# Summing v in the layout of its products, eight products on ScalarE, and rewritten orders up to the second tile

## The chip, the cores and the metric

One core of one Trainium2 chip. The metric is device time in microseconds of one execution of the whole program, the median of several runs. TensorE (PE) does matmuls and transposes, VectorE (DVE), ScalarE (ACT) and GpSimd (POOL) work on SBUF, SyncE (SP) issues DMAs. Each engine works through its own list in order and waits on semaphores.

## The reference

Inputs are q, k, v of shape (4 batches, 8 heads, 576 positions, 64) in fp32. The attention output is the sum of two parts:

```
pooled: q, k, v averaged over groups of 4 positions (144 rows), softmax attention over the 144, each row repeated 4 times
local:  scores of position i with |i - j| < 4 only (7 taps), softmax, times v
x = (pooled + local), reshaped to 2304 x 512
moe:  xn = x / rms(x) * g;  y = (silu(xn @ w_gate) * (xn @ w_val)) @ w_out      d_ff 1536
moe2: h = y @ w_in;  out = (s * relu(h)^2 + b) @ w_out                          d_ff 2048
```

## The kernel before, in words

The 576 groups of four positions are cut into five tiles `a` (or `t`) of up to 128 partitions; a partition holds four positions (`FAC`).

*Pooled attention* runs once for 4 x 8 = 32 heads `n`, in a pipeline over four engines: TensorE makes the scores (`CSC`, line 1480), VectorE the minimum `cneg` (line 1330; the scores come negated), ScalarE the exponents (`cs`, line 1168), TensorE turns them (line 1491), ScalarE copies them (`cpT`, line 1159), TensorE multiplies them with the summed v (`dv`, line 1513). TensorE works on score n, turn n-2 and product n-3 in one pass of its loop. Between passes it turns the summed q and k of the next batch (`turn_pooled`, line 1468; six units a batch, from the pass `UNIT_FROM` = 5 of the batch before). Their sums over four positions come first: q on VectorE (`pool_q`), k on GpSimd (`pool_k`). For v of batches 1 to 3, VectorE sums it in a layout of 128 partitions with nine rows each (`vd`); SP stores it to DRAM (`store_vd`) and loads it back with 72 partitions as `dv` (`load_dv`). Batch 0's v is already loaded with 72 partitions and summed there (`pool_v0`). `finish_pooled` scales the result by the inverse sum of the exponents, SP stores it (`store_co`) and loads it per tile (`load_ct`).

*Local attention* of a tile has 16 products in each of two phases, two for each head. In the first (`qk_mult`, line 532) GpSimd multiplies q with seven shifted windows of k, 128x896, and VectorE reduces over 64 (`qk_reduce`). After a softmax over seven taps on VectorE and ScalarE comes the second (`pv_mult`, line 546): GpSimd multiplies the probabilities with windows of v, writing with a stride of seven so that the taps lie side by side, and VectorE reduces over seven into `x` (`pv_reduce`). The products go through two buffers `prod`, so GpSimd is at most two products ahead of VectorE. Then the pooled part is added (`add_pooled0`, `add_pooled`), ScalarE squares and sums, VectorE finds the inverse root (Newton's steps), ScalarE scales x.

*First layer.* TensorE transposes x, ScalarE and VectorE split it into a high part, a low part and a bf16 copy (`split_hi`, `split_lo`, `split_bf`). Steps `s` of the layer: steps 0 to 11 are half a tile wide (256 columns), 12 to 17 full (512), together tile 0; then 12 steps for each further tile. A step is gate, value and, two steps later, output, 12 matmuls each, with `silu`, `hidden_mul`, `hidden_hi`, `hidden_lo` between them on ScalarE and VectorE. The weights come in 18 pieces through four buffers: load, high part on ScalarE (`weight_hi`), low part on GpSimd or VectorE (`weight_lo`).

*The order* is written out by hand. In each engine's loop over heads and, later, steps, tables say after which n or s a piece of tile 0's or tile 1's work stands (`QK0_AT`, `PV0_AT`, `SUMQ_AT`, `SUMV_AT`, `QK1_AT`, `PV1_AT`, `HI_AT`, `LO_AT`, `REST_AT`). SP's list of loads is one sequence. From tile 2 on the orders are common to before and after. Step 18 is the first of tile 1; its transposes stand after the output of step 14.

Of the kernel before, what the change touches and what calls it, by code (L numbers as in the profile page):

```python
# [4 lines left out]
F32 = mybir.dt.float32  # L5
# [3 lines left out]
ALU = mybir.AluOpType  # L9
# [61 lines left out]
HI_AT = {0: (6, 7), 2: (8,), 4: (9,), 5: (10,), 6: (11,), 8: (12,), 9: (13,), 10: (14,), 12: (15,), 13: (16,), 14: (17,)}  # L71
LO_AT = {0: (4,), 2: (6,), 4: (8,), 7: (10,), 9: (12,), 11: (14,)}
QK1_AT = {0: (7, 8), 1: (9,), 3: (10, 11), 4: (12,), 5: (13, 14), 6: (15,)}
PV1_AT = {8: (0, 1), 9: (2, 3), 10: (4, 5), 11: (6, 7), 12: (8, 9, 10, 11), 13: (12, 13, 14), 14: (15,)}

REST_AT = {("qk", 7): (5,), ("qk", 10): (7,), ("qk", 15): (9,), ("pv", 3): (11,), ("pv", 6): (13,), ("pv", 15): (15, 17)}

PRODUCTS = [("qk", 0, n) for n in range(16)] + [("pv", 0, n) for n in range(16)] + [("qk", 1, n) for n in range(16)]
# [26 lines left out]
QK_REST = {(1, 9): (2, 3), (1, 10): (4, 5, 6), (1, 11): (7, 8), (2, 0): (9, 10, 11, 12), (2, 1): (13, 14, 15), (3, 0): (13, 14, 15), (4, 0): (13, 14, 15)}  # L105
# [38 lines left out]

def build(nc, q, k, v, w_gate, w_val, w_out, rms_g, w2_in, w2_out, s2, b2, out):
    y_scr = nc.dram_tensor("y_scr", [TILES, P, DT, W_], F32, kind="Internal").ap()
    c_scr = nc.dram_tensor("c_scr", [G, E], F32, kind="Internal").ap()
    v_scr = nc.dram_tensor("v_scr", [B, H * J, D], F32, kind="Internal").ap()

    with ExitStack() as ctx:  # L150
# [81 lines left out]
        rawv = [None] + [place(at, f"rawv{b}", [P, QT, FAC * D], F32) for b in (1, 3)]  # L232
# [9 lines left out]
        rawv = [None, rawv[1], place(at, "rawv2", [P, QT, FAC * D], F32), rawv[2]]  # L242
# [66 lines left out]
        prod_ready, prod_used = sem("prod_ready"), sem("prod_used")  # L309
        shifted, expd, probs = sem("shifted"), sem("expd"), sem("probs")  # L310
# [80 lines left out]
        def weight_hi(act, n):  # L391
# [1185 lines left out]
```

## Time and profile before

| what | us |
|---|---|
| median of 3 runs | 1009.58 (1008.57 to 1010.66) |
| the profiled execution | 1014.44 |
| its span, first to last instruction | 1010.8 |
| busy: TensorE | 957.7 (95%) |
| busy: VectorE | 529.1 (52%) |
| busy: GpSimd | 416.6 (41%) |
| busy: ScalarE | 329.0 (33%) |

Busy shares are averages over stages with different limits: GpSimd has nothing left to do in the last third, and TensorE is not full in the first. The rows below are therefore taken by stage.

### The profile page before, as it was taken

The page shows a single profiled execution, that of the slowest core. Times are in us where ns is not written, and L with a number is a line of the kernel's source. Part 1 is how long each engine was busy: PE and PEld are TensorE (multiplying, and loading weights), DVE is VectorE, ACT ScalarE, POOL GpSimd, SP SyncE. Part 2 cuts the span into 40 slices and gives each one's busy share as a digit, 9 for nine tenths or more (in the row PEclk, how much of TensorE's full clock was granted, in tenths as well). Part 3 has the DMA queues.
Part 4 walks back from the last instruction along what each step waited for, and adds up shares of the span by engine and source line. Part 5 has one row for each costly group of instructions (what it writes and reads, how often), then busy time and mean ns, then how long its engine had stood idle before and what let it go on. Part 6 is the DMA issues. An engine that isn't in the chain of part 4 may idle for free.

```text
span 1010.8 us, 12761 instructions
## 1 busy us (share of the span) xinstructions
PE 957.7 (95%) x4836; PEld 766.2 (76%) x4864; DVE 529.1 (52%) x787; ACT 329.0 (33%) x704; POOL 416.6 (41%) x216
## 2 busy tenths in 40 slices
PE   4398899998999999999999999999999999999997
PEld 3276688966677777777777998888888888888896
DVE  4567878887676576555552223443433443433343
ACT  2244564425322431243123344322222322222232
POOL 4788889898787487555630255100000000000000
PEclk9999999999999999999999999999999999999999
DMA  9986345431422032102103243101001100100010
GB/s 255 276 250 194 102 134 159 151 110 51 137 72 82 21 121 75 41 19 71 32 7 125 83 127 105 42 1 64 21 0 42 42 1 1 63 1 1 0 43 21
DMA packets 54376, 79.38 MB, mean 79 GB/s; under 512 B 9836, under 2 KB 37068, under 8 KB 52908
## 3 DMA queue, kind: packets, MB, share of 16 engines
q1 hardware_dynamic: 53212, 73.86, 24.2%
q10 hardware_dynamic: 1104, 4.72, 1.2%
q8 instruction: 38, 0.62, 0.3%
q14 instruction: 22, 0.18, 0.1%
HBM read 67.05 MB, written 11.50 MB: 78 GB/s over the span
## 4 chain that ended last, share of the span: by engine, by line
PE 78%; POOL 7%; DVE 6%; issue 3%; ACT 2%; DMA 2%; SPq 1%; ACTq 0%; POOLq 0%; DVEq 0%
PE bank L727 23%; PE bank L867 7%; PE bank L868 6%; PE bank L869 6%; PE bank L849 6%; PE bank L850 6%; PE bank L851 6%; PE bank L763 4%; PE bank L761 4%; PE bank L762 4%; POOL prod L532 3%; POOL prod L546 2%; DMA rawk<-in_k_dram 2%; PE bank L1480 1%; DVE sc L552 1%
## 5 line engine op out<-in xcount | busy, mean ns | idle before, releaser
L532 POOL TENSOR_TENSOR prod<-qs,ks 128x896 f32<-128x896 f32 x80 | 177.2, 2238 | 73.4 <-DVE sc L552 61.0
L546 POOL TENSOR_TENSOR prod<-sc,vs 128x896 f32<-128x896 f32 x80 | 151.9, 2011 | 51.9 <-DVE x L562 32.5
L888 DVE SCALAR_TENSOR_TENSOR r<-bank,r 128x512 f32<-128x512 f32 (+1 forms) x80 | 51.0, 638 | 181.0 <-ACT r L876 181.0
L851 PE MATMUL bank<-y_h,w2i_l 128*128 128x512 f32 (+1 forms) x320 | 117.7, 368 | 0.0
L876 ACT ACTIVATE r<-bank 128x512 f32<-128x512 f32 (+1 forms) x80 | 44.4, 555 | 182.0 <-PE bank L851 181.2
L761 PE MATMUL bank<-h_h,wo_h 128*128 128x512 f32 (+1 forms) x264 | 102.7, 389 | 0.0
L552 DVE TENSOR_REDUCE sc<-prod 128x14 f32<-128x896 f32 x80 | 85.3, 1078 | 31.7 <-POOL prod L532 31.7
L783 DVE TENSOR_TENSOR bank<-bank,u 128x512 f32<-128x512 f32 (+1 forms) x66 | 39.5, 599 | 119.0 <-PE bank L727 119.0
L727 PE MATMUL bank<-x_h,wv_h 128*128 128x512 f32 (+1 forms) x264 | 100.4, 392 | 0.0
L562 DVE TENSOR_REDUCE x<-prod 128x128 f32<-128x896 f32 x80 | 85.8, 1079 | 18.0 <-POOL prod L546 17.4
L763 PE MATMUL bank<-h_h,wo_l 128*128 128x512 f32 (+1 forms) x264 | 93.2, 353 | 0.0
L762 PE MATMUL bank<-h_l,wo_h 128*128 128x512 f32 (+1 forms) x264 | 92.5, 350 | 0.0
L727 PE MATMUL bank<-x_l,wv_h 128*128 128x512 f32 (+1 forms) x264 | 90.8, 355 | 0.0
L727 PE MATMUL bank<-x_h,wg_h 128*128 128x512 f32 (+1 forms) x264 | 89.4, 360 | 1.0 <-ACT u L771 0.8
L727 PE MATMUL bank<-x_l,wg_h 128*128 128x512 f32 (+1 forms) x264 | 88.0, 355 | 0.3 <-DVE x_l L705 0.3
L867 PE MATMUL bank<-w2o_ha,g_h 128*128 128x512 f32 x216 | 84.3, 390 | 0.4 <-ACT y_st L797 0.4
L868 PE MATMUL bank<-w2o_la,g_h 128*128 128x512 f32 x216 | 84.2, 390 | 0.0
L869 PE MATMUL bank<-w2o_ha,g_l 128*128 128x512 f32 x216 | 84.0, 389 | 0.0
L882 ACT ACTIVATE g_h<-r 128x512 fp32r<-128x512 f32 (+1 forms) x80 | 47.1, 589 | 101.0 <-DVE r L890 101.0
L896 DVE TENSOR_TENSOR g_l<-r,g_h 128x512 fp32r<-128x512 f32 (+1 forms) x80 | 51.2, 639 | 52.5 <-ACT g_h L882 52.5
L777 ACT ACTIVATE h_h<-bank 128x512 fp32r<-128x512 f32 (+1 forms) x66 | 34.4, 521 | 133.1 <-DVE bank L783 133.1
L771 ACT ACTIVATE u<-bank 128x512 f32<-128x512 f32 (+1 forms) x66 | 34.3, 519 | 129.4 <-PE bank L727 129.3
(131 smaller groups left out, 1911.8 us busy)
## 6 DMA issues: line engine op xcount, KB each, us to landing
raww<-in_moe_w_out_dram SPq DMA_DIRECT2D x14, 512.0 KB, 3.9
ks<-in_k_dram SPq DMA_DIRECT2D x16, 280.0 KB
vs<-in_v_dram SPq DMA_DIRECT2D x16, 280.0 KB, 5.0
y_scr<-y_st ACTq DMA_DIRECT2D x4, 1024.0 KB, 4.0
raww<-in_moe_w_in_dram SPq DMA_DIRECT2D x8, 512.0 KB, 3.8
y_raw<-y_scr SPq DMA_DIRECT2D x4, 1024.0 KB, 4.9
out_dram<-o_st SPq DMA_DIRECT2D x16, 256.0 KB, 2.8
rawq<-in_q_dram SPq DMA_DIRECT2D x3, 1152.0 KB, 14.2
```

The costliest lines, as they stand in the source:

```text
L532: pool.tensor_tensor(dst, qv, kv, ALU.mult).then_inc(prod_ready, 1)
L546: pool.tensor_tensor(dst, pv, vv, ALU.mult).then_inc(prod_ready, 1)
L552: dve.tensor_reduce(sc[:, a % 2, n * 2 * BAND:(n + 1) * 2 * BAND], prod[:, at_ % 2, :].rearrange("p (s d) -> p s d", d=D), op=ALU.add, axi ...
L562: dve.tensor_reduce(x[:, 2 * half:2 * half + 2, h * D:(h + 1) * D], over(prod[:, at_ % 2, :], [[BAND * D, 2], [BAND, D], [1, BAND]]), op=A ...
L727: last = pe.matmul(o[:, 0:w], wt[:, m, kk, :], xs[:, kk, cols], start=i == 0, stop=i == 3 * DT - 1)
L761: pe.matmul(o, wo_h[:, m, cols], h_h[:, s % 3, 0:w], start=m == 0 and p != 1, stop=False)
L762: pe.matmul(o, wo_h[:, m, cols], h_l[:, s % 3, 0:w], start=False, stop=False)
L763: last = pe.matmul(o, wo_l[:, m, cols], h_h[:, s % 3, 0:w], start=False, stop=m == M1 - 1)
L851: last = pe.matmul(o, w2i_l[:, m, kk, :], y_h[t % 2][:, kk, 0:w], start=False, stop=kk == DT - 1)
L867: pe.matmul(o, g_h[:, r % 3, cols], wh[:, mh, :], start=m == 0, stop=False)
L868: pe.matmul(o, g_h[:, r % 3, cols], wl[:, mh, :], start=False, stop=False)
L869: last = pe.matmul(o, g_l[:, r % 3, cols], wh[:, mh, :], start=False, stop=m == M2 - 1)
```

## The change

- v of batches 1 to 3 is loaded in halves of 72 partitions (`load_rawv(b, g)`, three buffers) and summed where it is used, without `v_scr`: batches 1 and 2 on VectorE (`pool_v(b, g)`), batch 3 on GpSimd (`pool_v3(g)`).
- Four second-phase products of tile 0 and four of tile 1 (`ACT_PV`: n = 2, 6, 10, 13) go to ScalarE (`pv_taps`): for each of the product's two positions f seven ACTIVATEs, one a tap, of 128x64 with the probability as the per-partition scale, into a buffer `prod_a` of its own. VectorE reduces them with `pv_reduce_act`.
- `finish_pooled` is cut in two (`exponent_sums` and the scaling); `store_co` goes from SP's list to ScalarE's; `UNIT_FROM` becomes 4 for batches 2 and 3; the transposes of tile 0's second half go from steps 2 and 3 to 4 and 5.
- The orders of SP, GpSimd, VectorE and ScalarE up to step 17 are written as plain sequences. Waits change with the buffers: `weight_hi` of the first two pieces waits for two q sums and one k sum, `weight_lo` of the first four for v's sums, `split_hi` of the first chunk for `pool_v3`.

```diff
-UNIT_FROM = 5
+UNIT_FROM = {1: 5, 2: 4, 3: 4}
+ACT_PV = {0: (2, 6, 10, 13), 1: (2, 6, 10, 13)}
...
+        def pv_taps(act, a, n, f):
+            h, half = divmod(n, 2)
+            if f == 0:
+                act.wait_ge(probs, a + 1)
+                act.wait_ge(v_loaded[slot_of(a, h)], 48 * slot_turn(a, h))
+                wait(act, act_used, act_at(a, n))
+                if a == 1:
+                    act.wait_ge(co_stored, 16 * B)
+            for tap in range(BAND):
+                at_ = (h * FAC + 2 * half + f) * BAND + tap
+                last = act.activation(over(prod_a[a][:, f * BAND * D + tap:], [[BAND, D]]),
+                                      v_win(a, h)[:, (2 * half + f + tap) * D:(2 * half + f + tap + 1) * D],
+                                      ACT.Copy, scale=sc[:, a % 2, at_:at_ + 1])
+            if f == 1:
+                last.then_inc(act_made, 1)
...
+            def pool_v3(g):
+                i = 4 + g
+                rv = rawv[i % 3][0:JH, :, :]
+                pool.wait_ge(rawv_loaded[i % 3], 16 * (i // 3 + 1))
+                pool.wait_ge(cpv, H * (B - 3) + 4 * g + 4)
+                pool.tensor_tensor(rv[:, :, 0:2 * D], rv[:, :, 0:2 * D], rv[:, :, 2 * D:4 * D], ALU.add).then_inc(v_order, 1)
+                pool.wait_ge(v_order, g + 1)
+                pool.tensor_tensor(dv[0:JH, (B - 1) % 2, H * g:H * (g + 1), :], rv[:, :, 0:D], rv[:, :, D:2 * D], ALU.add).then_inc(v3_pooled, 1)
...
```

SP's new list, calls only, up to the second weight piece:

```
rawk0, rawq0 in thirds, load_rawv0(0), load_qk(0,0), load_rawq(1), load_qk(0,1), load_rawk(1), load_rawv0(1),
load_qk(0,2), load_rawv(1,0), load_qk(0,4), load_rawv(1,1), load_qk(0,3), load_rawq(2), load_rawk(2), load_qk(0,5),
load_rawv(2,0), load_v(0,0), load_qk(0,7), load_qk(0,6), small constants, load_rawv(3,0), load_rawq(3), load_rawk(3),
load_piece(0), load_v(0,1), load_rawv(2,1), load_rawv(3,1), load_qk(1,0), load_v(0,2), (0,4), (0,3), (0,5), load_ct(0), load_piece(1)
```

GpSimd's new list: `qk_mult(0, 0..3)`, `pool_k(1)`, `qk_mult(0, 4..9)`, `pool_k(2)`, `qk_mult(0, 10..15)`, `pool_v3(0)`, `pool_k(3)`, the `pv_mult` of tile 0 up to 14, `weight_lo(1)`, `pv_mult(0, 15)`, `qk_mult(1, 0)`, `weight_lo(0)`, `pool_v3(1)`, `qk_mult(1, 1..15)` with `weight_lo` 2, 5, 7, 9, 11, 13 among them, `qk_mult(2, 0)`, `qk_mult(2, 1)`, `weight_lo(15)`, the twelve `pv_mult` of tile 1.

VectorE's new list around the places that matter (`least` is the minimum of a head):

```
least 0, pool_v0(0), least 1, qk_reduce(0,0), least 2, 3, pool_q(1), qk_reduce(0,1), least 4, exponent_sums(0,0), least 5, qk_reduce(0,2), (0,3), pool_v0(1), ...
least 16, qk_reduce(0,14), pool_q(3), qk_reduce(0,15), least 17, softmax_max(0), least 18, 19, softmax_norm(0), least 20, pool_v(2,1), pv_reduce(0,0), ...
least 27, pv_reduce(0,14), add_pooled0(0), pv_reduce_act(0,13), pv_reduce(0,15), add_pooled0(1), qk_reduce(1,0), least 28, 29, inverse_root0, least 30, ...
```

ScalarE's new list: the half products of tile 0 stand between the exponents of heads 19 and 26, one or two a head; then `pv_taps(0,13,1)`, `squares0(0)`, `weight_hi(2)`, `keep_turned(25)`, `exponents(27)`, ... `squares0(1)`, ... `exponents(29)`, `normalise` of rows 0 and 1, `keep_turned(28)`, `store_co(2)`, `exponents(30)`, `keep_turned(29)`, `split_hi` of the first chunk. In tile 1 the half products stand between `silu(11)` and `hidden_hi(14)`.

## Rows read from the trace of the kernel before

**Rows 1.** Windows: length; busy PE, PEld, DVE, ACT, POOL (counts); PEclk, DMA share, GB/s

```profile
46.85:86.40 39.55, 34.61 (x191) 26.32 (x191) 30.20 (x44) 16.58 (x64) 31.57 (x16) 1.00 0.77 233
86.40:121.40 35.00, 31.56 (x180) 24.40 (x180) 28.11 (x35) 17.21 (x60) 29.60 (x17) 1.00 0.52 154
121.40:146.60 25.20, 23.23 (x143) 19.38 (x141) 18.66 (x35) 15.69 (x52) 21.25 (x10) 1.00 0.38 111
146.60:242.00 95.40, 90.72 (x595) 76.66 (x598) 77.98 (x103) 41.29 (x80) 84.44 (x39) 1.00 0.41 127
242.00:600.00 358.00, 356.13 (x1734) 266.85 (x1759) 193.51 (x276) 114.55 (x220) 200.38 (x99) 1.00 0.23 71
```

**Rows 2.** Chain that ended last, 9 to 48 us: start, us, what

```profile
12.06 18.43 DMA rawk<-in_k_dram
...
34.91 3.20 POOL prod L532 x2
...
42.04 2.22 DVE rawq L1283
...
44.28 2.52 DVE qd L1286
```

**Rows 3.** Timeline of TensorE: start, us, operation, [idle time before it]

```profile
46.85 0.85 PE L1468 MATMUL bank<-ident,qd 128*64 128x128 f32 x3 [16.46 <-DVE qd L1286]
...
88.65 1.23 PE L1480 MATMUL bank<-kT,qT 64*72 64x144 f32 x4
...
100.87 1.23 PE L1480 MATMUL bank<-kT,qT 64*72 64x144 f32 x4
...
140.01 1.94 PE L672 MATMUL bank<-ident,x 128*128 128x128 f32 x8 [1.64 <-ACT x L653]
...
146.60 1.20 PE L727 MATMUL bank<-x_h,wg_h 128*128 128x256 f32 x4
...
241.95 0.65 PE L672 MATMUL bank<-ident,x 128*128 128x128 f32 x4 [2.89 <-ACT x L653]
```

**Rows 4.** GpSimd's timeline, what follows the last second-phase products

```profile
121.28 2.37 POOL L413 TENSOR_TENSOR wg_l<-raww,wg_h 128x1024 bf16<-128x1024 f32 x1
...
227.28 2.41 POOL L413 TENSOR_TENSOR wv_l<-raww,wv_h 128x1024 bf16<-128x1024 f32 x1
```

**Rows 5.** The page, part 2: GB/s of the DMA engines in 40 equal slices

```profile
GB/s 255 276 250 194 102 134 159 151 110 51 137 72 82 21 121 75 41 19 71 32 7 125 83 127 105 42 1 64 21 0 42 42 1 1 63 1 1 0 43 21
```

**Rows 6.** Groups of GpSimd, 18 to 86 us. Count, busy us, mean ns, idle before

```profile
L532 POOL TENSOR_TENSOR prod<-qs,ks 128x896 f32<-128x896 f32 x16 | 36.8, 2327 | 10.9 <-DMA ks<-in_k_dram 5.6 <-DVE sc L552 5.3
L1102 POOL TENSOR_TENSOR kd<-kd,rawk 128x576 f32<-128x576 f32 x3 | 5.2, 1731 | 0.2
```

**Rows 7.** Groups of GpSimd, 121 to 242 us

```profile
L532 POOL TENSOR_TENSOR prod<-qs,ks 128x896 f32<-128x896 f32 x21 | 48.0, 2307 | 10.1 <-DVE sc L552 10.1
L546 POOL TENSOR_TENSOR prod<-sc,vs 128x896 f32<-128x896 f32 x17 | 34.0, 2096 | 4.8 <-DVE sc L552 3.6 <-DVE x L562 1.3
L413 POOL TENSOR_TENSOR wg_l<-raww,wg_h 128x1024 bf16<-128x1024 f32 x5 | 13.9, 2782 | 0.0
```

**Rows 8.** Groups of GpSimd, 86 to 122 us

```profile
L546 POOL TENSOR_TENSOR prod<-sc,vs 128x896 f32<-128x896 f32 x16 | 29.7, 1947 | 8.4 <-DVE x L562 5.4 <-DVE sc L591 3.0
```

**Rows 9.** Groups of ScalarE, whole span

```profile
L777 ACT ACTIVATE h_h<-bank 128x512 fp32r<-128x512 f32 x42 | 25.1, 598 | 88.0 <-DVE bank L783 88.0
L653 ACT ACTIVATE x<-x,rinv 128x512 f32<-128x512 f32 x20 | 12.9, 715 | 5.1 <-DVE rinv L636 5.1
L777 ACT ACTIVATE h_h<-bank 128x256 fp32r<-128x256 f32 x24 | 9.2, 385 | 45.1 <-DVE bank L783 45.1
```

**Rows 10.** ScalarE's timeline, the four scalings of tile 1's x

```profile
239.34 2.56 ACT L653 ACTIVATE x<-x,rinv 128x512 f32<-128x512 f32 x4 [5.14 <-DVE rinv L636]
```

**Rows 11.** DMA rate in two early stretches

```profile
14.00:20.00 6.00, 6.00 (x26) 4.77 (x26) 2.64 (x4) 2.45 (x10) 1.27 (x1) 1.00 1.07 231
20.00:26.00 6.00, 3.04 (x18) 2.25 (x16) 4.48 (x5) 1.34 (x8) 2.92 (x2) 1.00 1.02 321
```

More of the change, by code:

```diff
@@ L68 @@
     FIRST_ORDER += [("out", (_g + 1) * MH // 2 - 1)]
[L71 to L78, printed above, removed]
+ACT_PV = {0: (2, 6, 10, 13), 1: (2, 6, 10, 13)}
+PRODUCTS = [("qk", 0, n) for n in range(16)] + [("pv", 0, n) for n in range(16) if n not in ACT_PV[0]] + [("qk", 1, n) for n in range(16)]
 EARLY = {2: 2, 3: 4, 4: 4}
@@ L84 @@
         PRODUCTS += [("qk", _a + 1, n) for n in range(EARLY[_a + 1])]
-    PRODUCTS += [("pv", _a, n) for n in range(16)]
+    PRODUCTS += [("pv", _a, n) for n in range(16) if n not in ACT_PV.get(_a, ())]
 PLACE = {p: i for i, p in enumerate(PRODUCTS)}
@@ L1128, in _ @@
+            for a in range(2, TILES):
+                for n in range(EARLY[a], 16):
+                    qk_mult(pool, a, n)
                 if a + 1 < TILES:
@@ new lines, in _ @@
+            exponents(0)
+            exponents(1)
+            keep_turned(0)
+            exponents(2)
+            keep_turned(1)
+            exponents(3)
+            keep_turned(2)
+            exponents(4)
+            keep_turned(3)
+            exponents(5)
+            keep_pooled(1, 0)
+            keep_turned(4)
+            exponents(6)
+            keep_pooled(1, 1)
+            keep_turned(5)
+            exponents(7)
+            keep_pooled(1, 2)
+            keep_turned(6)
+            exponents(8)
@@ new lines, in _ @@
+            pv_taps(act, 1, 6, 1)
+            silu(act, 13)
+            pv_taps(act, 1, 10, 0)
+            pv_taps(act, 1, 10, 1)
+            hidden_hi(act, 13)
+            squares(act, 1, 0)
+            silu(act, 14)
+            pv_taps(act, 1, 13, 0)
+            pv_taps(act, 1, 13, 1)
+            hidden_hi(act, 14)
+            squares(act, 1, 1)
+            silu(act, 15)
+            hidden_hi(act, 15)
+            silu(act, 16)
+            normalise(act, range(FAC), 2)
+            hidden_hi(act, 16)
@@ L1199, in _ @@
+            split_hi(act, 2, 0)
+            split_bf(act, 2, 0)
+            silu(act, 17)
+            split_hi(act, 2, 1)
+            split_bf(act, 2, 1)
+            split_hi(act, 2, 2)
+            hidden_hi(act, 17)
+            split_bf(act, 2, 2)
+            split_hi(act, 2, 3)
+            split_bf(act, 2, 3)
+            for s in range(FIRST1, STEPS1):
                 p, m = STEP[s]
@@ L1359, in _ @@
-                if n == 31:
-                    qk_reduce(dve, 1, 2)
-            qk_reduce(dve, 1, 3)
+            for g in range(3):
+                pool_q0(g)
+            least(0)
+            pool_v0(0)
+            least(1)
+            qk_reduce(dve, 0, 0)
+            least(2)
+            least(3)
+            pool_q(1)
+            qk_reduce(dve, 0, 1)
+            least(4)
+            exponent_sums(0, 0)
+            least(5)
+            qk_reduce(dve, 0, 2)
+            qk_reduce(dve, 0, 3)
@@ L1370, in _ @@
+            split_lo(dve, 2, 2)
+            hidden_lo(dve, 17)
+            split_lo(dve, 2, 3)
+            qk_reduce(dve, 2, 7)
+            qk_reduce(dve, 2, 8)
+            for s in range(FIRST1, STEPS1):
                 p, m = STEP[s]
```

744 lines of the change are left out of this document (506 added, 238 removed).

## The prediction

> **What bounds the kernel now.** I read the busy shares by stage first, then the chain of waits, then TensorE's and GpSimd's timelines. The busy shares [rows 1] show one change of regime. From 242 us on TensorE is busy 356 of 358 us: whatever comes before is a head start that the rest keeps, one for one. Between 146.6 and 242 (tile 0 of the first layer) it is busy 90.7 of 95.4. Before 146.6 the 32 pooled heads and tile 0's window attention run, with TensorE, VectorE and GpSimd each 74 to 92% busy and none full. So I ask of the change only: when can tile 1's transposes, at 241.95 before, start?
>
> The chain [rows 2] says why the front is long: a DMA (k of batch 1, landed at 30.5), GpSimd's products behind it, VectorE's sum of q of batch 1 behind the reduces of these products, and only then TensorE's next transposes. TensorE stood 16.46 us for it [rows 3] and then ran heads nearly back to back: four in 12.2 us (88.65 to 100.87, two with q/k transposes and two without), 3.06 each. Step 0 starts at 146.60. Its tile ends at 239.06 (241.95 less the idle 2.89 before it), so tile 0 takes 92.5 us; TensorE then waits 2.89 for tile 1's x. GpSimd ends the second-phase products of tile 0 at 121.3 and those of tile 1 at 227.3 [rows 4]; from the latter to tile 1's transposes it is 14.7 us (reduce, add of the pooled part, squares, root, scaling).
>
> **The change part by part.**
>
> *Loads and orders up to the softmax of tile 0.* The sum of q of batch 1 now stands behind head 3 and one reduce, its load right behind window 0, the k load two transfers later. TensorE's stall at 30.4 to 46.85 therefore moves forward; what is late next is the transfers. Ahead of the last window needed, (0,6), the new order puts: q and k of batch 0 2.36 MB, v of batch 0 1.18, four loads of q or k 4.72, three v halves 1.77, eight windows 3.66, one v window 0.33, in all 14.0 MB. The page's rates per slice of 25.3 us [rows 5] move 6.44 MB by 25.3 and 13.4 by 50.5. When k of batch 1 landed, 7.9 MB had moved and 6.35 stood ahead of it in order, so 1.5 MB are in flight: (0,6) lands at 15.5 MB, 50.5 + 2.1/0.25 = 59 us; k of batch 2 (11.7 + 1.5) at 50. GpSimd: three k adds of 1.73 [rows 6], 50 to 55; products 10 to 15 at 2.33 [rows 6] end at 69; with 1.5 for VectorE's list, 70.5. Then come the half sum of v of batch 3 and k of batch 3 (5.2), which hide the softmax. The half sum is not in the trace: 72x1024 and 72x512 on GpSimd, nearest row the 128x1024 subtraction at 2.78 [rows 7], with half of it 4.2; by the k adds 1.73 x 1536/576 = 4.6; below, at the products' 1.95 for 896 [rows 8], 3.3. I take 4.2: the products of the second phase start at 80, against 86.4 before.
>
> *Four products on ScalarE.* GpSimd makes 12 instead of 16: 12 x 1.95 = 23.4 [rows 8]. One weight subtraction (2.78) now stands before the last of them, and I keep the 5.4 us of waits on reduces [rows 8] (the other 3.0 were the softmax): 31.6, against 35.0. The last product ends at 111.6 instead of 121.3. ScalarE gets 4 x 14 taps of 128x64 with a scale from memory. No such row exists. From the scaling of x, 0.715 at 512 columns with the same kind of scale, less 448 columns at (0.598 - 0.385)/256 = 0.83 ns [rows 9]: 0.34; four scalings took 2.56 instead of 2.86 [rows 10], so neighbours overlap by 0.10: 0.24 a tap, 13.4 us in all. The cover: ScalarE is busy 17.2 of 35.0 in that stage [rows 1], 17.8 are free. Ends: 0.1, were only the overlap and columns paid, and 0.715, no saving from the short row; I take 0.24, the row nearest in kind. VectorE's reduces stay 16. Its v sums shrink by the third batch and cost nothing new.
>
> *The waits that this adds on ScalarE.* The squares of rows 0 and 1 stand before head 27's exponents and wait for tile 0's add; heads 27 to 31 are queued behind. Twelve heads remain at the softmax, 12 x 3.06 = 36.7 behind 80, and about 4 for the lag of two or three heads: 121. Tile 0's x is later than that (below), so this queue costs nothing unless the heads slip by 5. The pooled result's stores go from SP's queue to ScalarE's; the third waits about 1 us for VectorE before head 30's exponents, also inside that 5. On SP the first weight piece waits for the last first-phase product and has v windows 1 to 7 behind it: 70.5 to 80 hides them, and without that cover it would cost some 5.
>
> *Step 0.* From the last product 14.7 us to the transposes, as tile 1 showed [rows 3, 4], then 6.6 to the first matmul [rows 3], of which transposes and split need about 3.5 (1.94 is the transposes' row) and the rest was heads in between; I take 5. Step 0 at 111.6 + 14.7 + 5 = 131.3. TensorE comes to tile 1 at 131.3 + 92.5 = 223.8.
>
> *Tile 1.* GpSimd from 111.6: 18 first-phase products (two of tile 2 now stand before the second phase) x 2.31 = 41.5, eight subtractions x 2.78 = 22.3, the other half sum 4.2, 12 second-phase products x 2.10 = 25.2 [rows 7]: 93.2. Before, by the same rows, 36.9 + 22.3 + 33.5 = 92.7 of the 106.0 between 121.3 and 227.3: the busy time does not shrink. Only the 13.3 of waits can, since tile 2's products and two subtractions fill the softmax (3.6 [rows 7]) and tile 1's first reduce no longer stands behind heads. I leave 4. Products end at 208.8, x is there at 208.8 + 14.7 = 223.5. Both arrive together, TensorE last.
>
> *Sum.* 241.95 - 223.8 = 18.2 us. The profiled execution took 1014.44, a span of 1010.8 and 3.6 around it, so 996.2 for it; the median of the runs shown is 1009.58, 4.9 lower, and the median is what is predicted: 991.4.
>
> **A rule against the change.** In 14 to 20 us, with the 72-partition v half in the queue, the DMA engines moved 231 GB/s at a share of 1.07; in 20 to 26 us 321 at 1.02 [rows 11]. The Trainium skill ("DMA: Bandwidth & Descriptors", section "Why a DMA increments its semaphore by 16 and not by 1") says that a transfer is spread over the largest number of engines up to 16 that divides its slowest dimension: for 72 partitions 12. By that, the three v halves ahead of window (0,6) cost a third more, 1.77/3/0.26 = 2.3 us, and the sum would be 993.7. The share in these rows is not the 0.75 that this would leave if nothing else moved, so the trace doesn't settle it.
>
> **Rivals.**
> *Tile 1 not earlier by more.* GpSimd's 13.3 us of waits in tile 1 stay, since VectorE's list still ties each reduce to a step of TensorE. For: VectorE is busy 78 of 95.4 there. Against: the two places named. x at 111.6 + 93.2 + 13.3 + 14.7 = 232.8, gain 9.1: 1000.5.
> *The front locks itself.* Each written order makes one engine's item wait for another's; the second phase starts at 86.4 as before. Step 0 at 86.4 + 31.6 + 19.7 = 137.7, tile 1 at 230.2, gain 11.7: 997.9.
> *Better.* The waits on reduces vanish and step 0 follows the heads at 124: tile 1 at 216.5, 984.
> *Slower: the taps on ScalarE.* They write with a stride of seven values and stand between the heads' exponents. Beyond 17.8/56 = 0.32 us each they no longer fit in the free time and hold heads 20 to 26, then the squares. At 0.64 each, 18 us over, the gain is gone; at 0.715 the front is 22 us later: 1013.6. For: no ScalarE row has such a destination. Against: GpSimd writes the second phase with the same stride at 1.95 and the first without it at 2.33 [rows 6, 8], so the stride is not dear there.
> *Nothing.* The transfers bound the front whatever the orders: within 2 us of before. Against: their share falls to 0.52 after 86.4 [rows 1].
>
> **How the numbers follow.** Under 0.2% (2 us) is what a measurement can't tell from no change. Forecast 0.55, own range 985 to 996; tile 1 0.15; the front's lock 0.12; better 0.07; taps 0.07; nothing 0.04. Faster 0.89, same 0.04, slower 0.07. The range 979 to 1002 leaves out the taps, nothing, the worse end of the two middle cases and the far end of the better one.
>
> **What would show it.** TensorE's long idle ends near 30, not 46.85; second-phase products start near 80 and end near 112; a tap takes about 0.34, 0.24 from start to start; step 0 near 131; tile 1's transposes near 224 with an idle under 2 before them; and from there the span as before. It is wrong if step 0 is early and tile 1's transposes still wait for x for several us, if ScalarE shows more than 0.3 a tap, or if heads 27 to 31 end after tile 0's x.

## The result and the profile after

The changed kernel takes 1005.04 us (median of 20 runs, 1002.41 to 1009.54) against 1010.14 for the kernel before in the same sessions (20 runs): a ratio of 0.9948, 95% interval 0.9935 to 0.9961. It is faster by about 5 us, where 18 were forecast, and its time lies outside the predicted range. The profiled execution took 1007.7 us with a span of 1005.6.

The stages of the changed kernel, cut where its own stages end, answer to [rows 1] (columns as there):

```profile
26.67:84.85 58.18, 50.02 (x274) 37.39 (x274) 48.61 (x57) 21.90 (x89) 48.10 (x24) 1.00 0.96 216
84.85:113.40 28.55, 26.20 (x145) 19.57 (x143) 25.07 (x32) 25.86 (x101) 25.20 (x14) 1.00 0.66 182
113.40:138.30 24.90, 15.18 (x96) 13.23 (x97) 22.75 (x32) 13.87 (x45) 17.35 (x9) 1.00 0.24 73
138.30:237.50 99.20, 94.05 (x600) 78.95 (x599) 77.75 (x104) 55.77 (x136) 81.07 (x36) 0.97 0.45 135
237.50:600.00 362.50, 361.34 (x1802) 271.00 (x1801) 193.50 (x276) 116.17 (x222) 199.64 (x99) 1.00 0.23 72
```

Read the lengths first. The second-phase products of tile 0 take 28.6 us instead of 35.0. The third stage, from the last of them to step 0, takes 24.9 us, as long as before (121.4 to 146.6), and TensorE is busy for only 15.2 of it, against 23.2: the equal length has another reason now. Tile 0 takes 99.2 us instead of 95.4, and its granted clock is 0.97. From tile 1 on nothing has changed: the span less the start of tile 1's transposes is 768.1 us, and was 768.8.

TensorE's timeline, answering to [rows 3]: transposes of q of batch 1, of x, step 0, two idles inside tile 0, and tile 1's transposes.

```profile
26.67 0.85 PE L1835 MATMUL bank<-ident,qd 128*64 128x128 f32 x3
...
131.86 1.94 PE L717 MATMUL bank<-ident,x 128*128 128x128 f32 x8 [7.12 <-ACT x L698]
138.32 0.99 PE L774 MATMUL bank<-x_h,wg_h 128*128 128x256 f32 x3
...
190.50 0.39 PE L774 MATMUL bank<-x_h,wv_h 128*128 128x256 f32 x1 [2.64 <-DVE h_l L836]
...
227.56 0.47 PE L774 MATMUL bank<-x_h,wg_h 128*128 128x512 f32 x1 [2.24 <-ACT u L818]
...
237.46 0.60 PE L717 MATMUL bank<-ident,x 128*128 128x128 f32 x4
```

The idle of 16.46 us is gone, as forecast. Against the forecast, each row from 131.86 on is late: x of tile 0 keeps TensorE idle for 7.12 us, two new idles stand inside tile 0, and tile 1 begins at 237.46 instead of 223.8, only 4.5 us earlier than before.

What is late at 131.86 stands on VectorE's timeline, in the inverse root of tile 0, 12 operations on 4 columns:

```profile
118.69 0.17 DVE L675 TENSOR_SCALAR var<-sqs 128x4 f32<-128x4 f32 x1
118.89 2.19 DVE L676 TENSOR_SCALAR halfv<-var 128x4 f32<-128x4 f32 x1
121.00 0.16 DVE L677 TENSOR_SCALAR rinv<-var 128x4 int32<-128x4 int32 x1
121.19 7.59 DVE L679 TENSOR_TENSOR newt<-rinv 128x4 f32<-128x4 f32 x1
128.81 0.16 DVE L680 TENSOR_TENSOR newt<-newt,halfv 128x4 f32<-128x4 f32 x1
```

Ten of the twelve last 0.16 or 0.17 us; one lasts 2.19 and one 7.59. GpSimd's timeline beside it:

```profile
118.71 2.35 POOL L1147 TENSOR_TENSOR rawv<-rawv 72x1024 f32<-72x1024 f32 x1
121.13 1.27 POOL L1149 TENSOR_TENSOR dv<-rawv 72x512 f32<-72x512 f32 x1
122.36 4.10 POOL L549 TENSOR_TENSOR prod<-qs,ks 128x896 f32<-128x896 f32 x2
126.42 2.34 POOL L426 TENSOR_TENSOR wg_l<-raww,wg_h 128x1024 bf16<-128x1024 f32 x1
134.32 2.07 POOL L549 TENSOR_TENSOR prod<-qs,ks 128x896 f32<-128x896 f32 x1 [5.56 <-DVE sc L594]
```

The operation of 2.19 us ends at 121.08, when GpSimd's instruction of 118.71 has ended (121.06); the one of 7.59 ends at 128.78, when the fourth of a row without a gap has ended (128.76). Then GpSimd itself idles 5.56 us, for a reduce that stands behind this root on VectorE. The kernel before had a small case of it that I read past: the first operation of the root took 2.01 us at 132.33, with GpSimd's products running until 134.32, and 0.17 at 327.90, with GpSimd idle.

```profile
130.21 4.11 POOL L532 TENSOR_TENSOR prod<-qs,ks 128x896 f32<-128x896 f32 x2
...
132.33 2.01 DVE L630 TENSOR_SCALAR var<-sqs 128x4 f32<-128x4 f32 x1 [1.66 <-ACT junk L618]
...
327.90 0.17 DVE L630 TENSOR_SCALAR var<-var 128x4 f32<-128x4 f32 x1
```

The two idles inside tile 0 cost more than themselves. Windows of the changed kernel behind each (columns as in [rows 1]):

```profile
190.50:194.50 4.00, 4.00 (x20) 3.72 (x21) 3.68 (x6) 3.69 (x16) 4.00 (x3) 0.57 0.00 0
...
227.50:232.00 4.50, 4.44 (x13) 2.68 (x14) 3.85 (x16) 0.60 (x1) 0.00 (x0) 0.62 0.02 5
```

The granted clock is 0.57 and 0.62 there, a mixture of the two levels 1.2 and 2.4 GHz, after 2.64 and 2.24 us in which TensorE stood; an estimate from these windows is some 1.7 us each of work not done (4.0 x 0.43, 4.5 x 0.38).

### The profile page after: what moved, and what is told of

Same layout as the page of the kernel before. It is cut to its first block, busy times and chain, and to the rows that moved or that the text cites. A ratio compares the mean times of both kernels' runs of the same rounds, so it can differ in the third digit from the quotient of the medians.

```text
span 1005.6 us, 12924 instructions
## 1 busy us (share of the span) xinstructions
PE 962.9 (96%) x4864; PEld 767.7 (76%) x4864; DVE 543.8 (54%) x790; ACT 354.8 (35%) x816; POOL 407.2 (40%) x211
## 4 chain that ended last, share of the span: by engine, by line
PE 77%; DVE 5%; POOL 4%; DMA 4%; SPq 3%; ACT 3%; issue 2%; ACTq 0%; DVEq 0%; POOLq 0%
PE bank L774 24%; PE bank L914 7%; PE bank L915 7%; PE bank L916 6%; PE bank L897 6%; PE bank L898 6%; PE bank L896 6%; PE bank L810 4%; PE bank L808 4%; PE bank L809 4%; POOL prod L549 3%; SPq L515 2%; ACT prod_a L576 1%; DMA rawv<-in_v_dram 1%; DMA ks<-in_k_dram 1%
## 5 line engine op out<-in xcount | busy, mean ns | idle before, releaser
L563 POOL TENSOR_TENSOR prod<-sc,vs 128x896 f32<-128x896 f32 x72 | 136.7, 2000 | 47.6 <-DVE x L604 29.0
L774 PE MATMUL bank<-x_l,wg_h 128*128 128x512 f32 (+1 forms) x264 | 88.2, 356 | 0.3 <-DVE x_l L752 0.3
L604 DVE TENSOR_REDUCE x<-prod 128x128 f32<-128x896 f32 x72 | 77.6, 1080 | 15.9 <-POOL prod L563 15.3
```

The costliest lines, as they stand in the source:

```text
L563: pool.tensor_tensor(dst, pv, vv, ALU.mult).then_inc(prod_ready, 1)
L604: dve.tensor_reduce(x[:, 2 * half:2 * half + 2, h * D:(h + 1) * D], over(prod[:, at_ % 2, :], [[BAND * D, 2], [BAND, D], [1, BAND]]), op=A ...
L774: last = pe.matmul(o[:, 0:w], wt[:, m, kk, :], xs[:, kk, cols], start=i == 0, stop=i == 3 * DT - 1)
```

## The experiments

Theory A: what was lost behind tile 0's products was lost because operations of VectorE's root cannot start while GpSimd runs without a gap. Beside it stood two other suspects: the order of VectorE's and ScalarE's lists inside tile 0 (the two idles), and the transfers of v ahead of the windows (second-phase products began at 84.85 instead of 80). The rivals: ScalarE's queue with the taps holds the heads and squares, or the front is bound by transfers alone.

All edits are to the changed kernel. Each ratio is to the kernel before, with its 95% interval; the changed kernel's is 0.9948. The table gives, from each profile, when the second-phase products of tile 0 begin and end, how far step 0 lies behind their end (the tail), how long tile 0 then takes to tile 1's transposes, and when these start.

| kernel | time us | ratio | products of tile 0 | tail | tile 0 | tile 1 at |
|---|---|---|---|---|---|---|
| forecast | 991.4 | | 80.0 to 111.6 | 19.7 | 92.5 | 223.8 |
| changed | 1005.04 | 0.9948 [0.9935, 0.9961] | 84.85 to 113.49 | 24.83 | 99.14 | 237.46 |
| e1 GpSimd held | 1001.18 | 0.9898 [0.9873, 0.9922] | 88.15 to 116.77 | 18.47 | 98.25 | 233.49 |
| e2 no taps | 1010.59 | 0.9992 [0.9978, 1.0006] | 84.74 to 118.09 | 24.82 | 97.89 | 240.80 |
| e3 two places | 1002.51 | 0.9908 [0.9887, 0.9928] | 83.43 to 112.05 | 24.83 | 94.56 | 231.44 |
| e4 e1 and e3 | 993.17 | 0.9840 [0.9819, 0.9861] | 82.41 to 111.05 | 18.47 | 92.45 | 221.97 |
| e5 v in two transfers | 1007.51 | 0.9976 [0.9962, 0.9990] | 85.30 to 114.81 | 24.81 | 97.08 | 236.70 |
| e6 root in PSUM | 1000.15 | 0.9907 [0.9887, 0.9927] | 81.27 to 109.91 | 20.02 | 98.32 | 228.25 |
| e7 e6 and e3 | 995.65 | 0.9865 [0.9844, 0.9887] | 87.32 to 115.96 | 20.02 | 92.53 | 228.51 |
| e8 v in 128 partitions | 1003.72 | 0.9936 [0.9917, 0.9955] | 81.03 to 109.65 | 24.84 | 97.46 | 231.95 |
| e9 e4, loads moved | 993.50 | 0.9835 [0.9817, 0.9853] | 84.06 to 112.69 | 18.47 | 92.65 | 223.81 |
| e10 first place alone | 1005.62 | 0.9955 [0.9940, 0.9970] | 82.23 to 110.87 | 24.84 | 98.43 | 234.14 |
| e11 second place alone | 1002.97 | 0.9932 [0.9913, 0.9952] | 83.57 to 112.21 | 24.82 | 95.25 | 232.28 |
| e12 smaller dose | 1003.39 | 0.9932 [0.9916, 0.9948] | 82.17 to 111.15 | 22.52 | 97.31 | 230.98 |

The tail repeats to 0.03 us in all seven kernels that leave the root and GpSimd's list beside it alone, so it is no chance of one profile; the start of the products does not repeat at all (81.3 to 88.2 in kernels with the same lists up to there). By their times alone e8, e10, e11 and e12 cannot be told from the changed kernel, since the intervals overlap; what they show, they show in the profiles. e2 and e5 are slower than the changed kernel, the others faster.

### The root: e1, e12, e6

```diff
             pool_v3(1)
+            pool.wait_ge(rinv_ready, 1)
             qk_mult(pool, 1, 1)
```

> The changed kernel, but GpSimd waits for tile 0's inverse root behind its second half sum of v of batch 3, before product 1 of tile 1. Theory A (the loss behind tile 0's products is VectorE's small operations of the root, which cannot start while GpSimd runs without a gap: one of 128x4 lasted 7.59 us and ended when GpSimd ended its fourth instruction): the long one lasts under 1.5 us, the root ends near 124 instead of 130.35, step 0 starts near 132 instead of 138.3, GpSimd loses 1.6 us at the wait and gets back the 5.6 us that it then waited for VectorE's reduce, tile 1's x and TensorE both come 4 to 6 us earlier: 999 to 1001. Rival (VectorE waited for something of its own, such as ScalarE's squares or the heads' exponents): the operation stays long, GpSimd only loses time, 1005 to 1009.

The long operation on VectorE, and GpSimd's instruction beside it:

```profile
124.46 1.23 DVE L679 TENSOR_TENSOR newt<-rinv 128x4 f32<-128x4 f32 x1
```

```profile
124.40 1.26 POOL L1149 TENSOR_TENSOR dv<-rawv 72x512 f32<-72x512 f32 x1
127.34 5.11 POOL L549 TENSOR_TENSOR prod<-qs,ks 128x896 f32<-128x896 f32 x2 [1.67 <-DVE rinv L681]
```

1.23 us instead of 7.59, to the end of the one instruction that still runs beside it. GpSimd pays 1.67 us at the wait and no longer idles 5.56. The tail falls by 6.36 us, the time by about 4. In this profile the products began 3.3 us later, so tile 1 starts only 3.97 earlier; where the products began in the other runs is not recorded. The rival is out: nothing of VectorE's list was changed, and the operation became short.

```diff
-            weight_lo(pool, 2)
             qk_mult(pool, 1, 3)
+            weight_lo(pool, 2)
```

> The changed kernel with one of GpSimd's four instructions beside the long operation of the root (a weight subtraction of 2.34 us, the last of the four) put behind the next product, which waits for VectorE. Theory A (the operation waits for the first gap of GpSimd): it lasts 7.59 less 2.34, 5.2 to 5.3 us, and step 0 comes 22.4 to 22.6 us behind the last product instead of 24.8; the time 1002 to 1004. Rival (the length comes from something else): 7.59 us as before.

The product that now stands ahead of the subtraction waits for VectorE, so the row without a gap is one instruction of 2.34 us shorter:

```profile
118.84 5.28 DVE L679 TENSOR_TENSOR newt<-rinv 128x4 f32<-128x4 f32 x1
```

```profile
120.01 4.09 POOL L549 TENSOR_TENSOR prod<-qs,ks 128x896 f32<-128x896 f32 x2
129.67 2.08 POOL L549 TENSOR_TENSOR prod<-qs,ks 128x896 f32<-128x896 f32 x1 [5.57 <-DVE sc L594]
```

7.59 less 2.34 is 5.25; 5.28 was measured, ending at 124.12 where GpSimd ends at 124.10. The tail is 22.52. Here the length of GpSimd's row decides the length of the wait.

The edit of e6, abridged:

```diff
-            a_link(dve, dve.tensor_scalar(var[:, c], var[:, c] if a else sqs[:, c], ...))
+            vr, rt = bank[5][:, 504:508], bank[5][:, 508:512]     # for tile 0; else var, rinv
+            a_link(dve, dve.tensor_scalar(vr, vr if a else sqs[:, c], ...))
...
-                a_link(dve, dve.tensor_tensor(newt[:, c], rinv[:, c], rinv[:, c], ALU.mult))
-                a_link(dve, dve.tensor_tensor(newt[:, c], newt[:, c], halfv[:, c], ALU.mult))
+                a_link(dve, dve.tensor_tensor(newt[:, c], halfv[:, c], rt, ALU.mult))
+                a_link(dve, dve.tensor_tensor(newt[:, c], newt[:, c], rt, ALU.mult))
```

> The changed kernel, but tile 0's root keeps its variance and its estimate in PSUM, so that no operation of it has two inputs or input and output in SBUF alone (save one product with one input in each); GpSimd waits for nothing more than before. Theory A (such operations of VectorE wait for a gap between GpSimd's instructions because both use one SBUF interface): all 12 operations last 0.2 to 0.25 us, the root takes 2.5 to 3 us instead of 11.7 although GpSimd runs on, transposes of x come some 12 us behind the last product instead of 18, step 0 near 131.5: 997 to 1000. Rival (any operation of VectorE waits while GpSimd runs back to back, or the loss has another cause): the long operations stay, 1004 to 1006.

Here GpSimd is not held. First and last operation of the root, and what GpSimd runs beside them:

```profile
115.10 0.17 DVE L679 TENSOR_SCALAR bank<-sqs 128x4 f32<-128x4 f32 x1
...
117.13 0.16 DVE L685 SCALAR_TENSOR_TENSOR rinv<-newt,bank 128x4 f32<-128x4 f32 x1
```

```profile
115.12 2.35 POOL L1151 TENSOR_TENSOR rawv<-rawv 72x1024 f32<-72x1024 f32 x1
117.55 1.27 POOL L1153 TENSOR_TENSOR dv<-rawv 72x512 f32<-72x512 f32 x1
```

The whole root lies inside 2.2 us, nearly all of it beside one GpSimd instruction of 2.35. So VectorE does not wait for GpSimd as such: with one operand in PSUM these operations, scalar and tensor ones alike, run beside it. The tail is 20.0 and not 18.5, because the same wait now meets the next operation on VectorE's list with both inputs in SBUF, a weight subtraction:

```profile
119.24 7.05 DVE L426 TENSOR_TENSOR wv_l<-raww,wv_h 128x1024 bf16<-128x1024 f32 x1
```

```profile
118.78 4.12 POOL L549 TENSOR_TENSOR prod<-qs,ks 128x896 f32<-128x896 f32 x2
122.86 2.35 POOL L426 TENSOR_TENSOR wg_l<-raww,wg_h 128x1024 bf16<-128x1024 f32 x1
```

It took 1.21 us at 131.67 in the changed kernel. Here it lasts until 126.29, 1.1 us behind the end of GpSimd's row (125.21). The minimum of the last head stands behind it on VectorE, that head's exponents behind the minimum on ScalarE, and TensorE waits 2.33 us at 127.57 for them. The time, 1000.15, is at the upper end of what was expected.

The wait is not always for the whole row. In tile 0 of the changed kernel the same kind of subtraction got in behind a single instruction, and GpSimd's next one then lasted 3.40 us (2.40 at 179.10):

```profile
153.52 2.13 DVE L426 TENSOR_TENSOR wo_l<-raww,wo_h 128x1024 fp32r<-128x1024 f32 x1
```

```profile
152.44 2.13 POOL L549 TENSOR_TENSOR prod<-qs,ks 128x896 f32<-128x896 f32 x1
154.51 3.40 POOL L426 TENSOR_TENSOR wo_l<-raww,wo_h 128x1024 fp32r<-128x1024 f32 x1
```

What decides between the two cases stays open.

### The two idles inside tile 0: e3, e10, e11

```diff
             hidden_mul(dve, 9)
-            weight_lo(dve, 14)
             qk_reduce(dve, 2, 0)
+            hidden_lo(dve, 9)
             softmax_norm(dve, 1)
-            hidden_lo(dve, 9)
...
             hidden_lo(dve, 11)
+            weight_lo(dve, 14)
             hidden_mul(dve, 12)
...
-            weight_hi(act, 16)
             hidden_hi(act, 9)
+            weight_hi(act, 16)
...
-            squares(act, 1, 1)
             silu(act, 15)
+            squares(act, 1, 1)
...
+            hidden_lo(dve, 14)
             add_pooled(dve, 1, 1)
-            weight_lo(dve, 16)
-            hidden_lo(dve, 14)
             hidden_mul(dve, 15)
+            weight_lo(dve, 16)
```

> The changed kernel with two places of tile 0 reordered: VectorE's residual of step 9 ahead of a weight subtraction and the softmax of tile 1; in step 15 ScalarE's silu ahead of the second squares and VectorE's residual of step 14 ahead of the add. Theory: TensorE's idles of 2.64 us (at 190.5) and 2.24 us (at 227.6) go, and with them the stretches at half clock behind them (about 2 us each), so TensorE is at tile 1 some 8 us earlier, near 229.5; but tile 1's x is ready near 235 as before, so TensorE now waits there and the gain is 2 to 3 us: 1002 to 1003. Rival (the half clock comes back at another place, or tile 1's x comes later because its operations were put behind): no gain, 1005.

Both idles are gone and tile 0 takes 94.56 us instead of 99.14. The time is as expected, but not for the reason given: TensorE does not wait ahead of tile 1's transposes (231.44, no idle before them); tile 1's x had come earlier too (ready at 230.64, and at 235.22 in the changed kernel).

The first hunks alone are e10, the last (from squares on) are e11.

> The changed kernel with the first of e3's two places alone (VectorE's residual of step 9 ahead of a weight subtraction and tile 1's softmax). If each idle of TensorE costs itself and a stretch at half clock behind it: the idle of 2.64 us at 190.5 goes with about 2 us of half clock, 4 to 5 us less for tile 0, 1000.5 to 1002.5. If the second place takes it all back: 1005.

> The changed kernel with the second of e3's two places alone (in step 15 ScalarE's silu ahead of the second squares, VectorE's residual of step 14 ahead of the add). The idle of 2.24 us at 227.6 and about 1.8 us of half clock go: 1001 to 1003; together with the first place's gain this should make the 2.5 to 5 us of e3. If tile 1's x is behind TensorE here: 1003 to 1005.

e10 brought next to nothing. Its second idle on TensorE:

```profile
223.21 0.77 PE L774 MATMUL bank<-x_h,wg_h 128*128 128x512 f32 x1 [3.89 <-ACT u L818]
```

It is 3.89 us instead of 2.24: counted from step 0, TensorE came to step 16 3.4 us earlier and waited there for the same silu, which came only 1.7 us earlier. It stood behind the squares, which stood behind tile 1's last sums. Another idle of 1.25 us had appeared at 210.83, also for a silu, and the granted clock behind the long idle was 0.50 for 4.5 us. So tile 0 became 0.7 us shorter. e11 alone shortened it by 3.9; its time is 2 us lower, which the intervals do not tell from the changed kernel. An idle earlier on a path is worth little while a later one holds the same engine for something that moves less.

The add ahead of these squares has both inputs in SBUF, and in the changed kernel it lasted 2.92 us from 221.85 on, beside a product of GpSimd that ended at 223.69, against 1.22 without one. So some 1.7 us of the way to that silu are the root's kind of wait again.

### Both together: e4, e7

> GpSimd's wait for the root (as in e1) and the two reordered places (as in e3) together. If the root's lock and the two stalls of TensorE are separate losses on one path, they add: e1 brought about 4 us and e3 about 2.5 to 5 against the changed kernel, so 996 to 999, tile 1's transposes near 228. If tile 1's x becomes the bound (products of tile 1 end near 213 to 216, x 14 us later), TensorE idles before tile 1's transposes and the time stays at 1000 to 1002.

e4 is the best kernel of the study, 993.17 us, faster than the changed kernel and than the one before. TensorE at x of tile 0, step 0 and tile 1:

```profile
123.06 1.94 PE L717 MATMUL bank<-ident,x 128*128 128x128 f32 x8 [0.77 <-ACT x L698]
...
129.52 1.20 PE L774 MATMUL bank<-x_h,wg_h 128*128 128x256 f32 x4
...
221.97 0.66 PE L717 MATMUL bank<-ident,x 128*128 128x128 f32 x4 [0.19 <-ACT x L698]
```

Tile 0 takes 92.45 us (92.5 forecast), tile 1 starts at 221.97 (223.8 forecast) with an idle of 0.19 for x: both arrive together. By the times the gains more than add: 3.9 and 2.5 us alone, 11.9 together, where 996 to 999 had been expected. In the profiles tail and tile 0 together are shorter by 7.2 us in e1, by 4.6 in e3 and by 13.0 in e4, which nearly adds; the starts of the products, which scatter by 7 us, may make up the rest of the times, but that is not shown. e3 also has two idles near 150 and 156 us (1.09 and 2.34) that e4 does not have. They do not follow the root: e9, with the same root and orders as e4, shows 1.13 and 0.52 at the same steps, and the changed kernel, with the long root, only one of 0.26. Their cause is open.

> The root in PSUM (as in e6) and the two reordered places (as in e3) together. If both losses are separate and GpSimd's list, now without a pause, keeps up: step 0 near 131.5, tile 0 in 93 to 95 us, tile 1's transposes near 225: 992 to 996, which is what the prediction had. If tile 1's x is the bound: 997 to 1000, with an idle of TensorE before tile 1's transposes.

e7 does as expected, 995.65, although its profile's front began 4.9 us later than e4's.

### The transfers: e5, e8, e9

The edits of e5 and e8, abridged:

```diff
-                sp.dma_start(rawv[i % 3][0:JH, :, :], ...).then_inc(rawv_loaded[i % 3], 16)
+                for p0, p1 in ((0, 64), (64, JH)):
+                    sp.dma_start(rawv[i % 3][p0:p1, :, :], ...).then_inc(rawv_loaded[i % 3], 16)
```

> The changed kernel, but each load of half a batch of v goes in two transfers, rows 0 to 63 and rows 64 to 71, instead of one of 72 rows. If a transfer of 72 rows is served by only part of the DMA engines: the stretch 26 to 38 us moves 260 to 290 GB/s instead of 190, GpSimd's wait of 6.1 us for window (0,3) shrinks by 2 to 4, second-phase products start near 81 instead of 84.85, and the time falls by 2 to 4 us: 1001 to 1003. If the rows do not matter: the rates and the start stay within 1 us, 1005.

```diff
+                sp.dma_start(rawv[i % 3][:, 0:4, :], 512 rows over 128 partitions).then_inc(...)
+                sp.dma_start(rawv[i % 3][:, 4, 0:2 * D], the other 64 rows, half a row each).then_inc(...)
```

> The changed kernel with the same 576 KB of each half batch of v of batches 1 to 3, loaded into 128 partitions of 4.5 rows instead of 72 of 8; the sums of v then run over the same shapes as before but over the wrong rows, so the pooled branch's values are not computed rightly here. If the rate of these transfers depends on how many partitions they end in: 26 to 38 us moves 260 to 300 GB/s instead of 190, GpSimd waits 2 to 4 us less for window (0,3), second-phase products start near 80 to 82 as predicted, the time is 2 to 4 us lower than the changed kernel's: 1001 to 1003. If not: rates and start as before, 1005.

The same two stretches of the kernel before, the changed kernel, e5 and e8 (columns as in [rows 1]; the last is GB/s):

```profile
26.00:32.00 6.00, 4.38 (x28) 3.70 (x28) 0.46 (x2) 1.38 (x6) 1.40 (x1) 1.00 0.97 277
32.00:38.00 6.00, 0.00 (x0) 0.00 (x0) 1.03 (x1) 0.00 (x0) 5.88 (x4) 1.00 1.06 306
```

```profile
26.00:32.00 6.00, 6.00 (x35) 4.42 (x33) 5.47 (x6) 2.45 (x11) 5.84 (x4) 1.00 0.94 186
32.00:38.00 6.00, 4.18 (x23) 2.96 (x23) 4.26 (x4) 2.69 (x11) 5.25 (x3) 1.00 1.04 196
```

```profile
26.00:32.00 6.00, 6.00 (x37) 4.72 (x36) 5.19 (x8) 2.56 (x12) 4.23 (x4) 1.00 1.12 178
32.00:38.00 6.00, 4.50 (x27) 3.29 (x25) 3.51 (x4) 1.69 (x7) 4.17 (x3) 1.00 1.12 180
```

```profile
26.00:32.00 6.00, 5.64 (x30) 3.83 (x28) 3.16 (x3) 1.28 (x5) 5.32 (x5) 0.50 1.12 237
32.00:38.00 6.00, 2.01 (x11) 1.39 (x11) 5.97 (x5) 2.60 (x11) 4.93 (x2) 0.50 1.12 269
```

With v in flight the rate is 186 to 196 GB/s at a DMA share near 1. Two transfers instead of one leave it at 178 to 180 with the share at 1.12; 128 partitions raise it to 237 and 269. GpSimd waited 6.12 us for window (0,3) and 2.48 for (0,6) in the changed kernel; in e8 no wait for a window over 1.5 us is left behind the first one. The time hardly follows: 0.9936 against 0.9948, with overlapping intervals. In this profile TensorE had the lower clock level from some 20 us to step 0 (0.50). That does not explain the small gain: eight of e8's twelve runs have such a mean clock (0.934 to 0.939), and at 1000.98 to 1005.84 us they are no slower than the other four (1001.12 to 1011.56). How much the 72 partitions cost in time stays open. The tail and tile 0 stood between it and the end in any case.

e5 missed both of its expectations: 1007.51 us, 2.5 above the changed kernel. Its profiled execution (1007.64) is as long as the changed kernel's (1007.7), so the profiles do not show where the two part.

```diff
-            load_qk(sp, 0, 4)
-            load_rawv(1, 1)
             load_qk(sp, 0, 3)
+            load_rawv(1, 1)
+            load_qk(sp, 0, 4)
...
-            load_qk(sp, 0, 7)
             load_qk(sp, 0, 6)
+            load_qk(sp, 0, 7)
```

> The kernel of e4 (GpSimd's wait for the root, both places reordered), and on SP's queue window (0,3) goes ahead of the second half of v of batch 1 and of window (0,4), and window (0,6) ahead of (0,7). If the front is bound by these arrivals (GpSimd waited 3.6 to 6.9 us for window (0,3) and up to 2.5 for (0,6)): second-phase products start near 79 to 80 instead of 82.4, and the time falls by 2 to 3 us to 990 to 991. If VectorE's written list holds GpSimd there anyway, or window (0,4) and q of batch 2 are late in turn: 993, or up to 2 us more.

No change (0.9835 against 0.9840): GpSimd no longer waits for window (0,3) but 2.94 us for a reduce at 42.51, so VectorE's written list holds it at the same place, and the products start no earlier (84.06).

### The taps: e2

The edit empties the two lists of products on ScalarE and puts the eight products and their reduces back into GpSimd's and VectorE's lists in numerical order.

```diff
-ACT_PV = {0: (2, 6, 10, 13), 1: (2, 6, 10, 13)}
+ACT_PV = {0: (), 1: ()}
```

> The changed kernel without the taps: the eight products go back to GpSimd, everything else (v in its products' layout, all orders) stays. By the working that a product on GpSimd costs 1.95 to 2.1 us and that ScalarE's taps lie beside other work: tile 0's products end 7 to 8 us later (near 121), step 0 later by the same less what the root's wait changes, tile 1's products 8 us later again: 1012 to 1020, slower than before the change, so the orders and the new v layout alone would give nothing. Rival (ScalarE's queue with the taps is what holds the heads and the squares): step 0 no later than 138.3 and 1003 to 1007.

Both expectations missed. The kernel without taps is as fast as the one before (0.9992), not slower: the products of tile 0 take 33.35 us instead of 28.64 and step 0 is 4.6 us later, but tile 1's transposes only 3.3, since tile 0 takes 97.89 us instead of 99.14. The rival is wrong as well: without the taps TensorE's wait for ScalarE's copy (3.58 us at 115.67) becomes longer, 5.60. So the whole measured gain of the change hangs on the taps; the new layout of v and all new orders brought nothing as long as the root and tile 0 gave it back.

## Why the prediction was wrong

**Point by point.** The long idle of TensorE moved as forecast: q of batch 1 is turned at 26.67. *Start of the second phase*: 80 forecast, 84.85 in the profile; ten profiles with the same lists up to there give 81.3 to 88.2, half of them below 83.5. In the profile GpSimd ended the sum of k of batch 2 at 57.85 instead of 55, behind 6.12 us of waiting for window (0,3); the half sum of v took 6.0 us instead of 4.2 (4.28 from 73.53 and 1.66 from 77.89); the softmax left 0.9 unhidden; the products behind that k took 0.4 more, the sum of the next k 0.8 less. The rate was mis-sized too, 0.25 to 0.26 MB per us forecast and 0.19 where v's halves moved, but e9, where that wait is gone, starts no earlier, so how much of the delay is the rate's is not shown. *The products*: 31.6 forecast, 28.64 measured; I had kept 5.4 us of waits on reduces, and 2.5 are left:

```profile
L563 POOL TENSOR_TENSOR prod<-sc,vs 128x896 f32<-128x896 f32 x12 | 23.0, 1988 | 3.4 <-DVE x L604 2.5 <-DVE sc L633 0.9
```

*A tap*: 0.24 from start to start forecast, and 14.8 us for 56 are 0.26 (each 0.41 long, 0.34 forecast):

```profile
L576 ACT ACTIVATE prod_a<-vs,sc 128x64 f32<-128x64 f32 x56 | 14.8, 409 | 0.3 <-DVE x L586 0.2
```

Together these put the last product at 113.5 instead of 111.6, a loss of 1.9.

**The step that failed first**: "From the last product 14.7 us to the transposes", with 5 more to step 0: 19.7 in all, 24.83 measured, 18.36 to the transposes and 6.46 from there. The 14.7 was taken from tile 1 as if it were a constant. The root in it already held two such waits, which the prediction read past:

```profile
233.05 2.15 DVE L647 TENSOR_TENSOR var<-sqs 128x4 f32<-128x4 f32 x1 [1.59 <-ACT junk L625]
235.23 2.03 DVE L630 TENSOR_SCALAR var<-var 128x4 f32<-128x4 f32 x1
```

```profile
233.06 4.17 POOL L532 TENSOR_TENSOR prod<-qs,ks 128x896 f32<-128x896 f32 x2
```

That is 3.9 us of waiting, against 9.4 in the changed kernel's root (2.19 and 7.59). The change put the second half sum of v, two products and a weight subtraction there without a gap. e1, e12 and e6 show that this is what cost it: held, 18.47; one instruction less, 22.52; operands in PSUM, 20.02. Of the 5.1 us missed, 1.5 are the 5, taken although the row before gave 6.6: two turns and four products of the last heads stand behind x's transposes on TensorE's list, as before, and e1 and e4, with the short tail, need the same 6.46. So the sign "heads 27 to 31 end after tile 0's x" came true without telling anything of the taps. The Trainium skill ("SBUF — State Buffer", section "SBUF: two separate sides") states the rule: the pair of SBUF interfaces that VectorE and GpSimd share is an exclusive lock between GpSimd's operations and those of VectorE with two SBUF inputs (against a GpSimd operation that reads SBUF, as all of these do) or in a two-port mode, and whichever starts first keeps it for the whole instruction. The traces agree, and go further: four instructions of GpSimd in a row kept it for 7.59 us.

**The step that failed second**: "tile 0 takes 92.5 us". 99.14 were measured, 4.9 of them the two idles and some 3.4 what the clock withheld behind them (the 92.5 held 1.8 us of idles of its own). I took the length of tile 0 from before although all orders inside it were written anew, and priced only GpSimd's list of tile 1. e3 gives 4.6 of it back, e3 and e1 together 6.7. The sum: 1.9 + 5.1 + 6.6 = 13.6 of the 13.7 us by which tile 1 was late.

**The rivals.** The measured gain, 5.1 us, lies between "nothing" (within 2) and "tile 1 not earlier by more" (9.1), nearer to the first in size; but the second phase's products ended 7.9 us earlier than before, so the transfers did not bound all. The premise of "tile 1 not earlier by more" held: from the last products of tile 0 to those of tile 1 GpSimd took 106.1 us, as before, not 97.2. But in the changed kernel TensorE was last, not x. In e4 the same way takes 98.5 and x is ready 0.19 us behind TensorE. The taps were no danger (e2). Whether the front locks itself is not settled: it began at 81.3 to 88.2, on both sides of the 86.4 named, and in e9 VectorE's list holds GpSimd; but the products, shorter than forecast, ended at 113.5 and not at 118. Step 0 came near that rival's 137.7 (138.3) by chance, through the root.

**The rule weighed in the prediction** (the Trainium skill, "DMA: Bandwidth & Descriptors", section "Why a DMA increments its semaphore by 16 and not by 1", 12 engines for 72 partitions) does not explain the rate: by it 64 of the rows on 16 engines should have been faster, and e5 moves 178 to 180 GB/s. Another page of the Trainium skill fits: "SBUF — State Buffer", section "Door 1: The DMA port swizzle (why `[64,N]` ≈ `[32,N]`)", by which partitions 0 to 63 reach only 8 of SBUF's 16 ports; it gives 196 GB/s for them and 328 for 128 partitions, each at 1 MiB. The stretches of 6 us here, with halves of v of 576 KB and other loads in flight, give 168 to 196 for 72 partitions and 237 to 346 for 128, so the sizes agree; that the ports are the reason is not tested by itself.

## What to carry to other kernels

Before work is moved on GpSimd, look at what small VectorE operations of the critical path will then run beside it, and at whether their operands lie in SBUF alone (reduces did not wait here): an operation of 0.16 us can take as long as GpSimd's row without a gap, and a wait on GpSimd, or operands in PSUM, buys it back. Then look at the next such operation on VectorE's list: in e6 the wait moved on to it. When lists inside a stage are written anew, its length is no constant to be carried over from before: each order in it needs its own pass over what stands ahead of each residual and activation. And a stall is worth its length only if no later one on the same path waits for something that moves less: e10 shortened tile 0 by 0.7 us for an idle of 2.64.

## What the runs showed that I had not expected

- A 128x4 operation of VectorE lasted 0.16, 1.23, 2.19, 5.28 and 7.59 us, and each of the last four ended within 0.03 us of the end of GpSimd's row. In the root it did not get in between GpSimd's instructions that followed each other without a gap. Elsewhere operations of VectorE did: at 153.52 in the changed kernel, and at 233.05 in the kernel before, between two products.
- Reduces do not wait: 128x896 took 1.07 us beside GpSimd throughout. The add of the pooled part, with both inputs in SBUF, does: in tile 1 it took 2.92 us from 221.85 on, GpSimd's products ending at 223.69, and 1.22 at 208.90.
- Stretches with loads into 72 partitions in flight moved 168 to 196 GB/s at a DMA share of 0.88 to 1.08, with the same bytes into 128 partitions 237 to 346 at 1.05 to 1.12.
- Identical lists begin the second phase anywhere from 81.3 to 88.2 us, while the tail behind it repeats to 0.03 us: a forecast of this front cannot be sharper than that. Why it scatters is not shown.
